# Two layers' matmuls as pairs of half-height products in one TensorE step

## The chip, the cores and the metric

The kernel runs on one core of one Trainium2 chip. The metric is the device time of one launch in microseconds (us), lower is better. TensorE is called PE (its weight loads PEld), VectorE DVE, ScalarE ACT, GpSimd POOL and SyncE SP.

## What is computed

A causal convolution over 7 taps per head (softmax of the taps first), then two feed-forward layers, each d_model 192, d_ff 2048, on 8192 tokens, float32 in and out.

```python
x = attn_out                                # conv of 7 taps over 2 x 4096 tokens, 192 channels
h = x @ w_in                                # layer 1
g = h * np.clip(h + 3.0, 0.0, 6.0) / 6.0
x = g @ w_out
h = x @ w_in2                               # layer 2
P = a[0] + a[1]*h + a[2]*h**2 + a[3]*h**3
Q = 1.0 + abs(b[0])*abs(h) + abs(b[1])*h**2
out = (P / (Q + 1e-6)) @ w_out2
```

## The kernel before

Tokens lie along the free dimension in 16 blocks of 512 (NB), d_ff in 16 tiles of 128 (NF), so each layer has 256 tiles (NT). To keep accuracy, each float32 operand is split in two fp32r parts, a rounded "hi" and a rest "lo". The 192 channels are kept as 128 (called a) and 64 (called b). Of b the hi and lo parts stand above each other in the 128 partitions of one tensor, `xb_hl`, so one matmul takes both.

**A tile's products.** `in_product` (line 359) makes h of one tile with five matmuls 128x512 into one PSUM bank: w_hi x a_hi, w_lo x a_hi, w_hi x a_lo, w_hi x b_hl, w_lo x b_hl. `out_product` (lines 371 to 377) adds one tile's g to the output sums with five: three into `ya_acc` (y0a_acc for layer 1, y1a_acc for layer 2 in the profile), then two into `yb_acc`, whose 128 rows hold the products of w_out's b columns, hi and lo part.

**The step.** An order written out by hand drives every engine. `course` lists steps; at step p PE does in1 of tile p (layer 1), in2 of tile s (layer 2, 21 tiles behind), out1 of tile p-2 and out2 of tile s-4: twenty matmuls. The table MIDDLE, with the lag of each operation, says in what order each other engine issues. ACT has eight operations a step: relu1 (writes r, line 463), rec2 (h<-rsq), sq2 (sqr), abs2 (den), lin2 (num), g1hi (g_hi<-r), g2hi (g_hi<-g), rsq2 (rsq). DVE has six: num2 (num, line 509), num1 (num, line 514), g_neg (g, line 569), gate1 (r<-r,h, line 470), newton (den, line 540), g_first (line 547). POOL has three: den_sum, g1lo, g2lo.

**Banks.** Eight PSUM banks: four for h, one each for the ya and yb sums of the two layers. From step 20 on all tiles of layer 1 use one h bank and those of layer 2 take turns in the three others. `wait_bank` makes PE wait: in1(p) for gate1(p-1), in2(s) for the third tile before it.

**Work once per block of 16 tiles.** The convolution's taps for later blocks (DVE, `conv_a_tap`, `conv_b_tap`), their split, and the hand-over from sums to inputs: when out1 of a block's last tile is done (n1_done), ACT copies y0a_acc (y1a_out) and rounds yb (`x2b_hi`), DVE makes the rest (`x2b_res`) and adds it to the lower-part sums (`x2b_lo`, which writes xb_hl of layer 2). The first out1 of the next block waits with its ya matmuls for y1a_out and with its yb matmuls for x2b_lo. In layer 2 the same holds for y2a_out (ACT) and `y2b_sum` (DVE, after y2b_move on ACT), which write the results that SP stores.

Of the kernel before, what the change touches and what calls it, by code (L numbers as in the profile page):

```python
# [11 lines left out]
P = 128  # L12
# [10 lines left out]
SUMS_READY, TAPS_READY = 5, 4  # L23


IN2, OUT1 = 20, 2


EARLY = IN2 + 1
# [96 lines left out]
def build_program(nc, x_a, x_b, taps, coefs, w_pack, out):  # L126
# [3 lines left out]
    NF = n_chunks * WCHUNK  # L130
# [3 lines left out]
    NT = NB * NF  # L134
# [7 lines left out]

    course, p, s = [], -1, -1
    while s < NT + SUM2 - NF + 1:
        one = p < NT + SUM1 - NF + 1
        p += one
        two = p >= IN2
        s += two  # L150
        course.append((p, s, one, two))
        if one and p in EXTRA:
            s += 1
            course.append((p, s, False, True))
# [28 lines left out]
    with ExitStack() as ctx:  # L183
# [13 lines left out]
        WO = DA + P + DA  # L197
        wout = [sb(f"wout{l}", NF * WO, F32R) for l in range(2)]
        stage_w = [sb(f"stage_w{i}", pack_cols) for i in range(W_STAGES)]

# [95 lines left out]
        def wait_buffer(eng, t, used, *others):  # L296
# [20 lines left out]
        names = """h1_done relu1 gate1 g1hi g1lo n1_done  # L317
# [44 lines left out]
        def out_product(eng, l, t, g_hi, g_lo, left):  # L362

            k, f = divmod(t, NF)
            c = f * WO
            w = wout[l]
            first, last = f == 0, f == NF - 1
            a_hi, b_hl, a_lo = w[:, c:c + DA], w[:, c + DA:c + DA + P], w[:, c + DA + P:c + WO]
# [8 lines left out]
            return eng.matmul(yb_acc[l][:, :], b_hl, g_lo[:, :], start=False, stop=last)  # L377


        def pe_in1(eng, t):  # L380
            split = ("cs_a_hi", "cs_a_lo", "cs_b_lo")
            if t < H_BANKS:
# [9 lines left out]
                in_product(eng, 0, t, h1_of(t), split, rest).then_inc(S["h1_done"], 1)  # L392
                return
            first_block_weights(eng, 0, t, "w_in_done")
            wait_bank(eng, 0, t)
            in_product(eng, 0, t, h1_of(t), split).then_inc(S["h1_done"], 1)

        def pe_out1(eng, t):
            first_block_weights(eng, 0, t, "w_out_done")
            eng.wait_ge(S["g1lo"], t + 1)  # L400
            out_product(eng, 0, t, g1_hi[t % 2], g1_lo[t % 2], ("y1a_out", "x2b_lo")) \
                .then_inc(S["n1_done"], 1)

# [13 lines left out]
        def pe_out2(eng, t):  # L417
            first_block_weights(eng, 1, t, "w_out_done")
            if t == 0:
                eng.wait_ge(S["g1lo"], EARLY)  # L420
            if t in full:
# [206 lines left out]
        def x2b_hi(eng, k):  # L628
            eng.wait_ge(S["n1_done"], (k + 1) * NF)
            after(eng, S["h2_done"], (k - 1) * NF)  # L630
            round_hi(eng, xb_hl[1][k % 2][0:DB, :], yb_acc[0][0:DB, :]).then_inc(S["x2b_hi"], 1)

        def x2b_res(eng, k):
            eng.wait_ge(S["x2b_hi"], k + 1)
            eng.tensor_tensor(x2b_rest[DB:P, :], yb_acc[0][0:DB, :], f32(xb_hl[1][k % 2][0:DB, :]),
                              ALU.subtract).then_inc(S["x2b_res"], 1)

        def x2b_lo(eng, k):
            eng.wait_ge(S["x2b_res"], k + 1)
            eng.tensor_tensor(xb_hl[1][k % 2][DB:P, :], x2b_rest[DB:P, :], yb_acc[0][DB:P, :],  # L640
                              ALU.add).then_inc(S["x2b_lo"], 1)


# [479 lines left out]
```

## Time and profile before

| | us |
|---|---|
| median of 2 runs | 1202.91 |
| profiled execution, time | 1202.42 |
| profiled execution, span of the instructions | 1200.3 |
| PE busy | 1185.5 |
| ACT busy | 1168.2 |
| DVE busy | 1157.7 |
| POOL busy | 1072.2 |
| PE weight loads busy | 962.9 |

Busy time is the union of an engine's instructions. Neighbouring instructions overlap at their ends, so an engine's rate is read from one start to the next. A row of the timeline gives start, duration, engine, line, operation, output <- inputs, shape, and in brackets idle time of the engine before it with what ended it.

### The profile page before, as it was taken

What the parts mean: (1) busy time and instruction counts of PE and PEld (TensorE: products, weight loads), DVE (VectorE), ACT (ScalarE), POOL (GpSimd) and SP (SyncE); (2) the same over time, 40 slices, a digit from 0 to 9 for tenths busy, and PEclk for the clock granted to TensorE, in tenths of its full rate; (3) what the DMA queues carried; (4) which work ended last, traced back from release to release, by engine and by line L of the source; (5) the groups of instructions that cost most, each with busy time, mean ns of one, the idle gap of its engine ahead of it and who ended that gap; (6) DMA issues with size and microseconds to landing.
All of it is one profiled execution on the core that took longest, in us unless ns stands there. A gap on an engine that the chain in (4) does not pass through costs nothing.

```text
span 1200.3 us, 18336 instructions
## 1 busy us (share of the span) xinstructions
PE 1185.5 (99%) x5145; PEld 962.9 (80%) x5145; DVE 1157.7 (96%) x1776; ACT 1168.2 (97%) x2235; POOL 1072.2 (89%) x829
## 2 busy tenths in 40 slices
PE   8999999999999999999999999999999999999988
PEld 6778888888888888888888888888888888888754
DVE  7899999999999999999999999999999999999898
ACT  8899999999999999999999999999999999999997
POOL 6889989999999989999899998999989999898875
PEclk9999999999999999999999999999999999999999
DMA  4400000000001000010000000000000000000010
GB/s 150 150 1 10 6 18 1 23 10 23 1 1 32 1 23 1 1 32 1 23 1 21 12 1 23 1 23 10 1 23 1 23 1 1 14 1 14 1 44 13
DMA packets 11317, 22.06 MB, mean 18 GB/s; under 512 B 1744, under 2 KB 3152, under 8 KB 11216
## 3 DMA queue, kind: packets, MB, share of 16 engines
q1 hardware_dynamic: 10928, 20.89, 5.9%
q8 instruction: 40, 0.66, 0.2%
q14 instruction: 61, 0.50, 0.1%
q10 hardware_dynamic: 288, 0.01, 0.0%
HBM read 14.60 MB, written 6.29 MB: 17 GB/s over the span
## 4 chain that ended last, share of the span: by engine, by line
PE 91%; ACT 4%; DVE 2%; issue 2%; POOL 0%; DMA 0%; ACTq 0%; DVEq 0%; POOLq 0%
PE h L359 45%; PE y0b_acc L376 5%; PE y0b_acc L377 5%; PE y0a_acc L371 5%; PE y0a_acc L373 5%; PE y0a_acc L372 5%; PE y1b_acc L377 4%; PE y1a_acc L373 4%; PE y1a_acc L371 4%; PE y1a_acc L372 4%; PE y1b_acc L376 4%; ACT rsq L524 0%; ACT g_hi L600 0%; ACT y0a_acc L536 0%; ACT num L491 0%
## 5 line engine op out<-in xcount | busy, mean ns | idle before, releaser
L520 POOL TENSOR_TENSOR den<-den,sqr 128x512 f32<-128x512 f32 x246 | 358.9, 1459 | 91.1 <-ACT den L497 90.1
L594 POOL TENSOR_TENSOR g_lo<-g,g_hi 128x512 fp32r<-128x512 f32 x246 | 321.7, 1308 | 5.3 <-ACT g_hi L600 5.3
L484 POOL TENSOR_TENSOR g_lo<-r,g_hi 128x512 fp32r<-128x512 f32 x235 | 306.9, 1306 | 5.5 <-ACT g_hi L600 3.6
L514 DVE SCALAR_TENSOR_TENSOR num<-num,coef,h 128x512 f32<-128x512 f32 x246 | 183.8, 747 | 8.3
L547 DVE SCALAR_TENSOR_TENSOR h<-num,coef,h 128x512 f32<-128x512 f32 x238 | 178.1, 748 | 0.2
L509 DVE TENSOR_TENSOR num<-num,h 128x512 f32<-128x512 f32 x246 | 167.8, 682 | 10.1 <-ACT num L491 3.9
L491 ACT ACTIVATE num<-h,coef 128x512 f32<-128x512 f32 x246 | 176.4, 717 | 0.2
L524 ACT ACTIVATE rsq<-den 128x512 f32<-128x512 f32 x246 | 159.0, 646 | 10.3 <-POOL den L520 7.2
L470 DVE SCALAR_TENSOR_TENSOR r<-r,h 128x512 f32<-128x512 f32 x235 | 160.7, 684 | 4.8 <-ACT r L463 3.7
L600 ACT ACTIVATE g_hi<-g 128x512 fp32r<-128x512 f32 x246 | 162.2, 659 | 2.4 <-DVE g L569 0.7
L540 DVE SCALAR_TENSOR_TENSOR den<-den,h 128x512 f32<-128x512 f32 x238 | 161.8, 680 | 0.6 <-ACT h L536 0.3
L569 DVE SCALAR_TENSOR_TENSOR g<-den,h 128x512 f32<-128x512 f32 x238 | 161.7, 679 | 0.2
L463 ACT ACTIVATE r<-h 128x512 f32<-128x512 f32 x256 | 154.4, 604 | 2.8 <-DVE y1b_acc L470 1.1
L600 ACT ACTIVATE g_hi<-r 128x512 fp32r<-128x512 f32 x235 | 156.3, 665 | 0.0
L497 ACT ACTIVATE den<-h 128x512 f32<-128x512 f32 x246 | 151.7, 617 | 1.7 <-DVE g L569 1.7
L503 ACT ACTIVATE sqr<-h 128x512 f32<-128x512 f32 x246 | 150.2, 610 | 0.6
L536 ACT ACTIVATE h<-rsq 128x512 f32<-128x512 f32 x240 | 147.4, 614 | 1.3
L371 PE MATMUL y0a_acc<-g_hi,wout 128*128 128x512 f32 x256 | 100.0, 390 | 2.2 <-DVE g_lo L484 1.6
L359 PE MATMUL h<-x0a_hi,win_hi 128*128 128x512 f32 x256 | 100.3, 392 | 1.1 <-DVE r L470 1.1
L359 PE MATMUL h<-x1a_hi,win_hi 128*128 128x512 f32 x256 | 100.5, 393 | 0.8 <-ACT x1a_hi L600 0.8
L359 PE MATMUL h<-x1a_lo,win_hi 128*128 128x512 f32 x256 | 99.7, 390 | 0.6 <-POOL x1a_lo L608 0.6
L359 PE MATMUL h<-x0a_lo,win_hi 128*128 128x512 f32 x256 | 99.6, 390 | 0.5 <-POOL win_lo L608 0.5
(177 smaller groups left out, 2995.9 us busy)
## 6 DMA issues: line engine op xcount, KB each, us to landing
stage_w<-w_pack SPq DMA_DIRECT2D x16, 448.0 KB, 3.3
raw_a<-x_a SPq DMA_DIRECT2D x16, 259.0 KB, 3.3
out<-y_a SPq DMA_DIRECT2D x16, 256.0 KB, 2.0
out<-y_b SPq DMA_DIRECT2D x16, 128.0 KB, 2.3
raw_b<-x_b SPq DMA_DIRECT2D x14, 129.5 KB, 2.7
r<-w_pack SPq DMA_DIRECT2D x4, 96.0 KB, 2.1
raw_b<-x_b SPq DMA_DIRECT2D x4, 65.5 KB, 4.7
y_a<-w_pack SPq DMA_DIRECT2D x2, 96.0 KB, 2.1
```

Of the source, the lines that this page charges most:

```text
L359: mm = eng.matmul(psum, w, x[:, :], start=(i == 0), stop=(i == len(passes) - 1))
L371: eng.matmul(ya_acc[l][:, :], a_hi, g_hi[:, :], start=first, stop=False)
L484: eng.tensor_tensor(g1_lo[t % 2][:, :], gated(t)[:, :], f32(g1_hi[t % 2][:, :]), ALU.subtract).then_inc(S["g1lo"], 1)
L491: eng.activation(num_of(t), h2_of(t), ACT.Identity, bias=a2, scale=reg_a3) \
L509: eng.tensor_tensor(n, n, h2_of(t), ALU.mult).then_inc(S["num2"], 1)
L514: eng.scalar_tensor_tensor(out=n, in0=n, scalar=a1, in1=h2_of(t), op0=ALU.add, op1=ALU.mult).then_inc(S["num1"], 1)
L520: eng.tensor_tensor(den_of(t), den_of(t), sqr_of(t), ALU.add).then_inc(S["den_sum"], 1)
L540: eng.scalar_tensor_tensor(out=den_of(t), in0=den_of(t), scalar=Q_ONE, in1=quotient(t), op0=ALU.add, op1=ALU.mult).then_inc(S["newton"], 1)
L547: eng.scalar_tensor_tensor(out=raw_quotient(t), in0=num_of(t), scalar=a0, in1=quotient(t), op0=ALU.add, op1=ALU.mult).then_inc(S["g_first" ...
L569: eng.scalar_tensor_tensor(out=g2[t % 2][:, :], in0=den_of(t), scalar=2.0, in1=raw_quotient(t), op0=ALU.subtract, op1=ALU.mult) \
L594: eng.tensor_tensor(g2_lo[t % 2][:, :], g2[t % 2][:, :], f32(g2_hi[t % 2][:, :]), ALU.subtract).then_inc(S["g2lo"], 1)
L600: return eng.activation(dst, src, ACT.Copy)
```

## The change

For the 232 steps that have tiles of both layers in full (p from 24 to 255), `pe_step` takes the place of the four calls. A matmul is cut in two halves of 64 contraction rows (partitions 0 to 63 and 64 to 127). `side_by_side` issues two halves behind each other that use different rows of the array and different banks: one of layer 1, one of layer 2. The groups follow one another: five pairs with layer 1's lower and layer 2's upper rows of the in products; the two yb pairs of the out products; four pairs with the in products' other rows (the fifth, w_lo x the b_lo rows of `xb_hl`, is not issued); three ya pairs; then the out products' other rows, two yb and three ya pairs. That is nineteen pairs. PE waits for its own earlier half before it writes the same bank from the other rows. Both layers' h are done behind the eleventh pair, both out products at the end of the step.

For the upper and lower rows to fit, layer 2's input b now holds its lo part in partitions 0 to 63 and hi in 64 to 127 (`x2b_hi`, `x2b_res`, `x2b_lo` write other partitions), and layer 1's w_out has its b columns first, lo before hi. For layer 1's odd blocks, whose `xb_hl` has hi in the upper rows, the product that is not issued is w_lo x b_hi. The orders of ACT, DVE, POOL and SP are what they were.

```diff
+        def side_by_side(eng, one, two, rows1, rows2, starts=(False, False), stops=(False, False)):
+            (out1, w1, x1), (out2, w2, x2) = one, two
+            return (eng.matmul(out1, w1[rows1, :], x1[rows1, :], start=starts[0], stop=stops[0]),
+                    eng.matmul(out2, w2[rows2, :], x2[rows2, :], start=starts[1], stop=stops[1]))
+        def pe_step(eng, p, s, n):
+            lower, upper = slice(0, DB), slice(DB, P)
+            t1, t2 = p - OUT1, s - OUT2
...
+            wait_bank(eng, 0, p)
+            wait_bank(eng, 1, s)
...
+                mm = side_by_side(eng, one, two, lower, upper, (i == 0, i == 0))
+            mm[0].then_inc(S["h1_part"], 1)
+            mm[1].then_inc(S["h2_part"], 1)
+
+            eng.wait_ge(S["g1lo"], t1 + 1)
+            eng.wait_ge(S["g2lo"], t2 + 1)
+            eng.wait_ge(S["n1_done"], t1)
+            after(eng, S["n2_done"], t2)
...
+            mm = first_rows((3, 4), ("x2b_lo", "y2b_sum"))
+            mm[0].then_inc(S["y1b_part"], 1)
+            mm[1].then_inc(S["y2b_half"], 1)
+
+            eng.wait_ge(S["h1_part"], n)
+            eng.wait_ge(S["h2_part"], n)
+            for i, (one, two) in enumerate(ins[:4]):
+                mm = side_by_side(eng, one, two, upper, lower, stops=(i == 3, i == 3))
+            mm[0].then_inc(S["h1_done"], 1)
+            mm[1].then_inc(S["h2_done"], 1)
+
+            mm = first_rows((0, 1, 2), ("y1a_out", "y2a_out"))
+            mm[0].then_inc(S["y1a_part"], 1)
+            mm[1].then_inc(S["y2a_half"], 1)
+
+            eng.wait_ge(S["y1b_part"], n)
+            eng.wait_ge(S["y2b_half"], n)
+            for i in (3, 4):
+                side_by_side(eng, *outs[i], upper, lower, stops=lasts if i == 4 else never)
+            eng.wait_ge(S["y1a_part"], n)
+            eng.wait_ge(S["y2a_half"], n)
+            for i in (0, 1, 2):
+                mm = side_by_side(eng, *outs[i], upper, lower, stops=lasts if i == 2 else never)
+            mm[0].then_inc(S["n1_done"], 1)
+            mm[1].then_inc(S["n2_done"], 1)
...
-            round_hi(eng, xb_hl[1][k % 2][0:DB, :], yb_acc[0][0:DB, :]).then_inc(S["x2b_hi"], 1)
+            round_hi(eng, xb_hl[1][k % 2][DB:P, :], yb_acc[0][DB:P, :]).then_inc(S["x2b_hi"], 1)
...
+        if not packs:
+            o = np.concatenate([o[:, :, da:], o[:, :, :da]], axis=2)
```

The first place is PE's step up to the end of h1. Before (h is layer 1's bank with x0 inputs, layer 2's with x1), the middle of a step's in products:

```order
L359 MATMUL h<-x0b_hl,win_hi 128x512
L359 MATMUL h<-x0b_hl,win_lo 128x512
L359 MATMUL h<-x1a_hi,win_hi 128x512 [waits g_done]
L359 MATMUL h<-x1a_hi,win_lo 128x512
L359 MATMUL h<-x1a_lo,win_hi 128x512
```

h of layer 1 is complete with the second row, the fifth matmul of the step. Now, the pairs of the upper and lower rows with which both h are completed:

```order
L412 MATMUL h<-x0a_hi,win_hi 128x512 [waits h2_part,h1_part]
L413 MATMUL h<-x1a_hi,win_hi 128x512
L412 MATMUL h<-x0a_hi,win_lo 128x512
L413 MATMUL h<-x1a_hi,win_lo 128x512
L412 MATMUL h<-x0a_lo,win_hi 128x512
L413 MATMUL h<-x1a_lo,win_hi 128x512
L412 MATMUL h<-x0b_hl,win_hi 128x512
L413 MATMUL h<-x1b_hl,win_hi 128x512
L412 MATMUL y0a_acc<-g_hi,wout 128x512 [waits y1a_out]
```

These are the eighth to eleventh pair; h of layer 1 moved from the fifth matmul behind the eleventh pair.

The second place is PE at the first tile of a block of layer 1, the out product's waits. Before:

```order
L359 MATMUL h<-x1b_hl,win_hi 128x512
L359 MATMUL h<-x1b_hl,win_lo 128x512
L371 MATMUL y0a_acc<-g_hi,wout 128x512 [waits y1a_out,g1lo]
L372 MATMUL y0a_acc<-g_hi,wout 128x512
L373 MATMUL y0a_acc<-g_lo,wout 128x512
L376 MATMUL y0b_acc<-g_hi,wout 128x512 [waits x2b_lo]
L377 MATMUL y0b_acc<-g_lo,wout 128x512
```

The wait for x2b_lo stands thirteen matmuls into the step. Now:

```order
L412 MATMUL h<-x0b_hl,win_lo 128x512
L413 MATMUL h<-x1b_hl,win_lo 128x512
L412 MATMUL y0b_acc<-g_hi,wout 128x512 [waits n2_done,n1_done,x2b_lo,g2lo,g1lo]
L413 MATMUL y1b_acc<-g_hi,wout 128x512
L412 MATMUL y0b_acc<-g_lo,wout 128x512
L413 MATMUL y1b_acc<-g_lo,wout 128x512
L412 MATMUL h<-x0a_hi,win_hi 128x512 [waits h2_part,h1_part]
```

It stands five pairs into the step, ahead of the other half of both h. There are 14 such rows with x2b_lo, and 14 with y2b_sum in its place.

The third place is DVE at the same step, where x2b_lo (line 640) is released. It reads the same before and now, but for the line numbers:

```order
L547 SCALAR_TENSOR_TENSOR h<-num,coef,h 128x512 [waits rec]
L509 TENSOR_TENSOR num<-num,h 128x512 [waits sq2,lin2]
L635 TENSOR_TENSOR x2b_rest<-y0b_acc,x1b_hl 64x512 [waits x2b_hi]
L640 TENSOR_TENSOR x1b_hl<-x2b_rest,y0b_acc 64x512 [waits x2b_res]
L514 SCALAR_TENSOR_TENSOR num<-num,coef,h 128x512 [waits num2]
L569 SCALAR_TENSOR_TENSOR g_0<-den,h 128x512 [waits g2lo,g_first,newton]
L470 SCALAR_TENSOR_TENSOR r_0<-r_0,h 128x512 [waits relu1]
```

Nothing moved on DVE.

## Rows read from the trace of the kernel before

**Rows 1.** The page: span, busy time of the engines, chain that ended last

```profile
span 1200.3 us, 18336 instructions
...
PE 1185.5 (99%) x5145; PEld 962.9 (80%) x5145; DVE 1157.7 (96%) x1776; ACT 1168.2 (97%) x2235; POOL 1072.2 (89%) x829
...
PE 91%; ACT 4%; DVE 2%; issue 2%; POOL 0%; DMA 0%; ACTq 0%; DVEq 0%; POOLq 0%
```

**Rows 2.** Window 600 to 750: busy (xcount) of PE, PEld, DVE, ACT, POOL, clock, DMA

```profile
600.00:750.00 150.00, 150.00 (x663) 124.20 (x662) 147.54 (x226) 148.06 (x284) 137.62 (x104) 1.00 0.04 12
```

**Rows 3.** Timeline, a step without block work on ACT and DVE

```profile
340.91 0.68 DVE L470 SCALAR_TENSOR_TENSOR r<-r,h 128x512 f32<-128x512 f32 x1
...
341.03 0.58 ACT L503 ACTIVATE sqr<-h 128x512 f32<-128x512 f32 x1
...
344.11 0.60 ACT L463 ACTIVATE r<-h 128x512 f32<-128x512 f32 x1
...
344.75 0.69 DVE L470 SCALAR_TENSOR_TENSOR r<-r,h 128x512 f32<-128x512 f32 x1
...
345.11 0.61 ACT L503 ACTIVATE sqr<-h 128x512 f32<-128x512 f32 x1
```

**Rows 4.** Timeline, block work on ACT and one tap on DVE

```profile
338.35 0.62 ACT L614 ACTIVATE y_a<-y0a_acc 128x512 f32<-128x512 f32 x1
338.82 0.66 ACT L524 ACTIVATE rsq<-den 128x512 f32<-128x512 f32 x1
...
339.82 0.67 ACT L600 ACTIVATE x1a_hi<-y_a 128x512 fp32r<-128x512 f32 x1
340.49 0.60 ACT L536 ACTIVATE h<-rsq 128x512 f32<-128x512 f32 x1
...
640.40 0.74 DVE L700 SCALAR_TENSOR_TENSOR conv_a<-raw_a,tap,conv_a 128x512 f32<-128x512 f32 x1
641.06 0.75 DVE L547 SCALAR_TENSOR_TENSOR h<-num,coef,h 128x512 f32<-128x512 f32 x1
```

**Rows 5.** Timeline, PE's weight loads behind a wait and in the stream

```profile
17.80 0.19 PEld L371 LDWEIGHTS y0a_acc<-g_hi,wout 128*128 128x128 f32 x1 [1.25 <-POOL wout L608]
17.91 0.19 PEld L372 LDWEIGHTS y0a_acc<-g_hi,wout 128*128 128x128 f32 x1
...
337.06 0.19 PEld L359 LDWEIGHTS h<-x0a_hi,win_lo 128*128 128x128 f32 x1
...
341.65 0.19 PEld L359 LDWEIGHTS h<-x0a_hi,win_hi 128*128 128x128 f32 x1 [0.32 <-DVE r L470]
...
341.75 0.19 PEld L359 LDWEIGHTS h<-x0a_hi,win_lo 128*128 128x128 f32 x1
```

**Rows 6.** Timeline, first tile of a block of layer 1, from the gate before it

```profile
334.98 0.69 DVE L470 SCALAR_TENSOR_TENSOR r<-r,h 128x512 f32<-128x512 f32 x1
...
337.06 0.39 PE L359 MATMUL h<-x0a_hi,win_hi 128*128 128x512 f32 x1
...
337.35 0.61 ACT L600 ACTIVATE x1b_hl<-y0b_acc 64x512 fp32r<-64x512 f32 x1
...
338.21 0.68 DVE L635 TENSOR_TENSOR x2b_rest<-y0b_acc,x1b_hl 64x512 f32<-64x512 f32 x1
...
338.93 0.69 DVE L640 TENSOR_TENSOR x1b_hl<-x2b_rest,y0b_acc 64x512 fp32r<-64x512 f32 x1
...
340.00 0.39 PE L376 MATMUL y0b_acc<-g_hi,wout 128*128 128x512 f32 x1
```

**Rows 7.** Timeline, first tile of a block of layer 2, from the gate before it

```profile
362.35 0.68 DVE L470 SCALAR_TENSOR_TENSOR r<-r,h 128x512 f32<-128x512 f32 x1
...
364.46 0.39 PE L359 MATMUL h<-x0a_hi,win_hi 128*128 128x512 f32 x1
...
366.25 0.68 DVE L660 SCALAR_TENSOR_TENSOR y_b<-y1b_acc,y_b 64x512 f32<-64x512 f32 x1
...
368.54 0.39 PE L376 MATMUL y1b_acc<-g_hi,wout 128*128 128x512 f32 x1
```

More of the change, by code:

```diff
@@ L23 @@
 SUMS_READY, TAPS_READY = 5, 4
-IN2, OUT1 = 20, 2
+IN2, OUT1, OUT2 = 20, 2, 4
 EARLY = IN2 + 1
@@ L151, in build_program @@
         course.append((p, s, one, two))
+        if one and two and p < NT and s >= OUT2:
+            in1_both.add(p)
+            in2_both.add(s)
+            out1_both.add(p - OUT1)
+            out2_both[s - OUT2] = (p, s, len(out2_both) + 1)
         if one and p in EXTRA:
@@ L315, in build_program @@
         d_const, d_tap, d_out_a, d_out_b = (sem(n) for n in ("d_const", "d_tap", "d_out_a", "d_out_b"))
-        names = """h1_done relu1 gate1 g1hi g1lo n1_done
+        names = """h1_done h1_part h2_part y1a_part y1b_part y2a_half y2b_half relu1 gate1 g1hi g1lo n1_done
                    h2_done lin2 abs2 sq2 num2 num1 den_sum rsq_done rec newton g_first g_done less_two g_gpsimd
@@ L367, in out_product @@
             first, last = f == 0, f == NF - 1
[L368 removed]
+            a_hi, b_hl = w[:, c + OUT_A[l]:c + OUT_A[l] + DA], w[:, c + OUT_B[l]:c + OUT_B[l] + P]
+            a_lo = w[:, c + DA + P:c + WO]
             if first:
@@ L377, in out_product, with in_places @@
             return eng.matmul(yb_acc[l][:, :], b_hl, g_lo[:, :], start=False, stop=last)
+        def in_places(l, t, psum):
+            k, f = divmod(t, NF)
+            par, c = k % 2, f * 2 * P
+            hi, lo = win_hi[l], win_lo[l]
+            return [(psum, hi[:, c:c + P], xa_hi[l][par]), (psum, lo[:, c:c + P], xa_hi[l][par]),
+                    (psum, hi[:, c:c + P], xa_lo[l][par]), (psum, hi[:, c + P:c + 2 * P], xb_hl[l][par]),
+                    (psum, lo[:, c + P:c + 2 * P], xb_hl[l][par])]
@@ new lines, in pe_step, with first_rows @@
+        def pe_step(eng, p, s, n):
+            lower, upper = slice(0, DB), slice(DB, P)
+            t1, t2 = p - OUT1, s - OUT2
+            ins = list(zip(in_places(0, p, h1_of(p)), in_places(1, s, h2_of(s))))
+            outs = list(zip(out_places(0, t1, g1_hi[t1 % 2], g1_lo[t1 % 2]),
+                            out_places(1, t2, g2_hi[t2 % 2], g2_lo[t2 % 2])))
+            wait_bank(eng, 0, p)
+            wait_bank(eng, 1, s)
+            needs = {0: ("cs_a_hi", "x2a_hi"), 2: ("cs_a_lo", "x2a_lo"), 3: ("cs_b_lo", "x2b_lo")}
+            for i, (one, two) in enumerate(ins):
+                for t, name in zip((p, s), needs.get(i, ())):
+                    if t % NF == 0:
+                        eng.wait_ge(S[name], t // NF + 1)
+                mm = side_by_side(eng, one, two, lower, upper, (i == 0, i == 0))
[5 more added lines that the diff above has]
+            after(eng, S["n2_done"], t2)
+            starts, lasts = (t1 % NF == 0, t2 % NF == 0), (t1 % NF == NF - 1, t2 % NF == NF - 1)
+            never = (False, False)
+            def first_rows(part, left):
+                for i in part:
+                    for t, start, name in zip((t1, t2), starts, left):
+                        if start and i == part[0]:
+                            after(eng, S[name], t // NF)
+                    mm = side_by_side(eng, *outs[i], lower, upper, starts if i == part[0] else never)
+                return mm
+            mm = first_rows((3, 4), ("x2b_lo", "y2b_sum"))
[20 more added lines that the diff above has]
+            mm[1].then_inc(S["n2_done"], 1)
@@ L394, in pe_in1 @@
             first_block_weights(eng, 0, t, "w_in_done")
+            if t in in1_both:
+                return
             wait_bank(eng, 0, t)
@@ L399, in pe_out1 @@
             first_block_weights(eng, 0, t, "w_out_done")
+            if t in out1_both:
+                return
             eng.wait_ge(S["g1lo"], t + 1)
@@ L405, in pe_in2 @@
             first_block_weights(eng, 1, t, "w_in_done")
+            if t in in2_both:
+                return
             wait_bank(eng, 1, t)
@@ L420, in pe_out2 @@
                 eng.wait_ge(S["g1lo"], EARLY)
+            if t in out2_both:
+                pe_step(eng, *out2_both[t])
+                return
             if t in full:
```

21 lines of the change are left out of this document (16 added, 5 removed).

## The prediction

> **What bounds the kernel now.** The page's first part comes first [rows 1]: TensorE (PE) is busy 99%, ScalarE (ACT) 97%, VectorE (DVE) 96% of a span of 1200.3 us, and the chain of waits runs 91% over PE. The stretch 600 to 750 says the same of the middle: 663 matmuls in 150 us, so one per 226.6 ns, and a step of twenty in 4.53 us, with no idle PE [rows 2]. So PE is the bound, but how near are the others? A busy share hides that here, because neighbouring instructions overlap; I read from start to start. The timeline of 341 to 346 us holds a step without block work: ACT's eight operations take 4.08 us from one sqr to the next, DVE's six 3.84 us from one r to the next [rows 3]. To that comes the work done once per block of 16 steps, priced by the start of the next instruction: some 8.5 operations of ACT at 0.47 to 0.67 us (4.6 us), and some 13 of DVE at 0.66 to 0.72 (8.7 us) [rows 4, 6]. That makes 4.08 + 4.6/16 = 4.37 us of ACT and 3.84 + 8.7/16 = 4.38 us of DVE per step. Both have only 3% less to do than PE. The profiled execution took 1202.42 us (1200.3 us and 2.1 around it), the median of the runs is 1202.91, the same thing; I sum against 1202.4.
>
> **What the change takes from PE.** 232 steps (those with tiles of both layers) go from 20 full matmuls to 38 half ones in 19 pairs; the rest of the program, 505 matmuls, stays. If a pair costs what one matmul costs, a step takes 19 x 0.2266 = 4.31 us, 0.23 less, and 52 us could go in all. The trace has no matmul on half of the rows, so I bound the pair. From below: 226.6 ns, since both halves stream 512 columns. From above: both halves one after the other, 453 ns. What could hold it between is the weight load, of which a pair has two. A load lasts 188 ns, but the second of two starts 0.11 us after the first where nothing holds it [rows 5], so two take 0.22 us of the load path and just fit into 0.2266. I take 226.6 ns as the nearest row, without margin: 0.24 is easily possible.
>
> A load starts as the matmul before it starts, in the same rows of the array (337.06 both) [rows 5, 6], so it loads under a running matmul. Next to that stands a rule. The Trainium skill ("TensorE: Matmul & The Clock Gate", Part 3, What overlaps and what doesn't) says that a weight load overlaps matmuls in flight only when its row group differs. By that rule each half would take its load and its matmul in turn; the trace of the full array disagrees, and what it would cost is part of rival (c).
>
> **The loop through the single h bank of layer 1.** h1 of step p+1 may start only when gate1(p) is done. Before, h1 is finished by the fifth of twenty matmuls; now by the eleventh of nineteen pairs (the order rows of the first place). Counted from a step's first matmul T: the eleventh starts at T + 2.27, ends 0.39 later [rows 6], and with 0.04 for the signal (as between relu1's end and gate1 [rows 3]) relu1 starts at T + 2.70. gate1 starts 0.64 after relu1 and takes 0.68, the first weight load follows 0.06 after it and the next one, with which the stream is under way, 0.11 after that [rows 3, 5]. The sum is 4.19 us, under 4.31, so the loop alone does not bind. But its slack has gone from over 1.2 us to 0.12: before, gate1 ends 1.39 us ahead of the next step (334.98 + 0.69 against 337.06) [rows 6]; now at most 0.3. Before, that slack lets ACT and DVE be late by a block operation and catch up. Now a step is about the largest of PE's 4.31, ACT's 4.08 and DVE's 3.84, each with its own block work in that very step. DVE with one tap has 4.50, ACT with one block operation 4.6. For the 14 of 16 steps that are not boundaries (below) this gives 4.50 us where nothing is evened out, and 4.33 where all is. I take 4.45, nearer to the first: 0.08 less than now, over 204 steps -17 us.
>
> **The waits at the block's boundary.** This is the step that decides. PE's out product of the first tile of a block may not overwrite y0b_acc before DVE's x2b_lo has read it, nor y1b_acc before y2b_sum. Before, the yb product stands after the ya product, thirteen matmuls into the step (layer 1) and eighteen (layer 2). In the change the yb pairs come first, right behind five pairs, at T + 1.13 (order rows, second place). In the trace x2b_lo ends at 338.93 + 0.69 = 339.62, T + 2.56, with T = 337.06 and PE needing it at 340.00 [rows 6]. y2b_sum ends at 366.25 + 0.68 = 366.92, T + 2.46, needed at 368.54, T + 4.08 [rows 7]. ACT's and DVE's order is unchanged (the order rows of the third place stand so in both), so even with the phase of before PE would stop 1.4 us. And the phase moves: gate1(p-1) ended 1.39 and 1.43 us ahead of T, now 0.17 to 0.3, so DVE stands some 1.15 us later against PE [rows 6, 7]. The release comes at T + 3.7. Then PE has to load (0.17), run the two yb pairs and the four upper pairs (the last starts 1.13 later), and the loop goes on: relu1 1.74 us after the release, gate1 at 2.38, the next step at 3.23. The step lasts 3.7 + 3.2 = 6.9 us in place of 4.53. The order shows 14 such places for x2b_lo and 14 for y2b_sum: 28 x 2.37 = +66 us. What covers nothing here: the second halves of h1 and h2 stand behind the waiting yb pair, and relu1, gate1, sq2 behind these. The floor of such a release is what hangs on n1_done: the last matmul of the step before ends at about T + 0.2, then x2b_hi 0.61, x2b_res 0.68, x2b_lo 0.69, T + 2.3 [rows 6]; then the step would be 5.5 us.
>
> **Edits with no price.** PE's waits for its own sums (h1_part, y1b_part, y1a_part) keep the two halves of one bank apart. Two of the three stand two pairs behind what they wait for: a matmul ends 0.39 after its start, signal and load make 0.17 of it more, 0.56, and the next pair is due at 0.68, so with the second half starting 0.11 late nothing is left. I put them at zero; if they show, 0.1 each, twice in 232 steps, +46 us at most, less where PE waits for gate1 anyway. x2b's swapped rows are the same instructions on DVE and ACT, and the weights' new order costs one different slice. g1lo and g2lo are needed 1.2 and 2.3 us earlier in the step and have two and four steps of lag.
>
> **Sum.** 1202.4 - 17 + 66 = 1252 us.
>
> **Rivals.**
> (a) Faster, or even: the boundary costs its floor and all else is evened out. 28 x 0.97 = +27, 204 x 0.20 = -41: 1188 us. To be over 2% faster the boundary would have to cost nothing, against [rows 6]. For it: the stop lets ACT and DVE work off what they are behind with. Over 2% faster 0.04, within 2% (up to 1227, boundary at its floor and the rest near 4.45) 0.13.
> (b) A pair costs more than one matmul: 0.25 us, by two loads of 0.11 and the 0.03 that lies between a matmul's start and the end of the load's turn. PE's step is 4.75, the loop 4.4: 204 x 0.25 = +51, 28 x 2.8 = +78: 1331 us. Chance 0.12. The Trainium skill ("TensorE: Matmul & The Clock Gate", Part 3) gives 3.07 times for four row tiles in place of four; that speaks for a pair dearer than one matmul, and no row here shows it.
> (c) The halves are not side by side (the change does not do what it says): 38 x 0.2266 = 8.61 us, 232 x 4.08 = +946, 2150 us. A load that waits for its own rows' matmul (0.11 + 0.39 = 0.50 us per pair) is dearer still: 19 x 0.50 = 9.5 us, 2355 us. Chance of both 0.05. The second is what the page's rule on row groups above would give.
> (d) The clock: PE would stand still 2.7 us in 28 places; the granted clock is 1.00 in the middle [rows 2], and the longest stop before, once PE runs, is 1.25 us [rows 5]. If it fell from 2.4 to 1.2 GHz after each stop and the next 4 us (my guess) went at half the rate, 28 x 2 = +56: 1308 us. Chance 0.06.
>
> **Numbers.** The forecast's own case has 0.60. The predicted time is 1252. The range goes from 1212 (shift of the phase half as large, the rest at 4.40) to 1290 (pairs of 0.24 us or the own waits showing): it leaves out (c), most of (b) and (d), and the good end of (a). 2% is about what a measurement tells from no change: under 1179 faster, over 1227 slower. Faster 0.05, within 14%, slower 0.81.
>
> **What the next profile would show.** Right: PE's time per pair 0.227 from start to start; 28 steps of nearly 7 us, with PE waiting over 2 us for x1b_hl and y_b of DVE; a few tenths of waiting for DVE's r in most other steps; DVE and ACT busy shares down to 92 to 94%. Wrong: pairs of 0.24 or more (b), no overlap of the two halves (c), a clock under 1.00 (d), or a wait for y_b under 1.5 us (a). What would upset the whole is a wait that PE has on itself and that I priced at nothing.

## The result and the profile after

The changed kernel takes 1303.44 us (median of 2 runs, 1302.61 to 1304.28) against 1202.91: 1.084 times the time of before, 95% interval 1.079 to 1.088. The prediction had the direction and the main mechanism, 1252 us and a range up to 1290; the loss is 100 us where it had 49. The profiled execution took 1304.28 us, 101.9 more than that of before.

The page of the changed kernel, its span, busy line, chain shares and three groups (name and shape, xcount | busy, mean ns | idle before, releaser):

```profile
span 1302.2 us, 28016 instructions
...
PE 1201.0 (92%) x9321; PEld 996.0 (76%) x9321; DVE 1167.4 (90%) x1776; ACT 1183.6 (91%) x2235; POOL 1071.0 (82%) x829
...
DVE 31%; PE 31%; ACT 22%; issue 14%; POOL 1%; ACTq 0%; DMA 0%; DVEq 0%; POOLq 0%
...
L412 PE MATMUL y0b_acc<-g_hi,wout 64*128 64x512 f32 x464 | 186.2, 401 | 70.4 <-DVE y_b L766 35.5
L576 DVE SCALAR_TENSOR_TENSOR r<-r,h 128x512 f32<-128x512 f32 x235 | 161.2, 686 | 88.3 <-ACT r L569 86.5
L569 ACT ACTIVATE r<-h 128x512 f32<-128x512 f32 x256 | 153.0, 598 | 86.9 <-PE h L412 78.5
```

Against [rows 1], the chain is no longer one engine's: PE's share has gone from 91% to 31%, and DVE, ACT and issue hold the rest. That is the picture of a loop that passes through three engines. PE stands idle 70.4 us in front of the first yb pair, and gate1 (DVE, line 576) and relu1 (ACT, line 569) wait in their turn, since the second halves of h stand behind that pair.

The windows of the changed kernel (columns as in [rows 2]): the middle, and then four of 2 us around one stop.

```profile
600.00:750.00 150.00, 137.75 (x1148) 113.99 (x1146) 136.49 (x208) 137.49 (x260) 126.92 (x95) 0.98 0.05 12
122.00:124.00 2.00, 0.05 (x2) 0.08 (x2) 1.94 (x4) 1.95 (x4) 2.00 (x3) 1.00 0.00 0
124.00:126.00 2.00, 2.00 (x12) 1.87 (x14) 1.06 (x2) 0.13 (x1) 0.72 (x1) 0.64 0.00 0
126.00:128.00 2.00, 2.00 (x12) 1.83 (x12) 0.69 (x1) 1.57 (x4) 0.38 (x1) 0.51 0.00 0
128.00:130.00 2.00, 2.00 (x21) 1.96 (x19) 1.71 (x3) 2.00 (x5) 1.81 (x2) 1.00 0.00 0
```

PE is idle from 122 to 124, and then the granted clock, the last column but two, reads 0.64 and 0.51: PE is at its lower level, 1.2 GHz in place of 2.4, for about 3.4 us in all, and a window of 2 us holds 12 half matmuls instead of 21. ACT and DVE are busy for only 1.7 and 1.75 us of these 4, since they wait for PE, so this time is lost to the whole loop. Before, no stretch up to PE's last matmul reads under 1.00. Counted in windows of 2 us, the changed kernel has 21 such stretches: behind all 14 waits for y2b_sum, behind 6 of the 14 for x2b_lo, and one at 1240, in the last part.

The pairs, from PE's timeline of the changed kernel, with the load of one (rows in order of start):

```profile
603.97 0.39 PE L413 MATMUL h<-x1a_hi,win_lo 64*128 64x512 f32 x1
...
604.03 0.39 PE L412 MATMUL h<-x0a_hi,win_lo 64*128 64x512 f32 x1
604.03 0.18 PEld L412 LDWEIGHTS h<-x0a_lo,win_hi 64*128 64x128 f32 x1
604.21 0.39 PE L413 MATMUL h<-x1a_lo,win_hi 64*128 64x512 f32 x1
...
604.26 0.39 PE L412 MATMUL h<-x0a_lo,win_hi 64*128 64x512 f32 x1
...
604.43 0.39 PE L413 MATMUL h<-x1b_hl,win_hi 64*128 64x512 f32 x1
```

Two halves start 0.06 us apart, the next two 0.23 later: a pair costs one full matmul. The load of 604.03 runs under a matmul of layer 1 that occupies the same 64 rows, so in this kernel too a load overlaps a matmul of its own row group. The Trainium skill ("TensorE: Matmul & The Clock Gate", Part 3, What overlaps and what doesn't) says that a load overlaps matmuls in flight only when its row group differs; these rows disagree with it.

**The step lengths**, from the first matmul of one step to that of the next, account for the loss; values for several steps are means. The description of the step gives layer 2 a lag of 21 tiles; it is 20 up to step 235 and 19 after it, which only says which steps hold the waits for y2b_sum.

| steps of the 232 | before | after | difference, us |
|---|---|---|---|
| 14 with the wait for x2b_lo | 4.53 | 7.12 at full clock | +36 |
| 14 with the wait for y2b_sum | 4.53 | 7.30 at full clock (from e2 and e4) | +39 |
| the clock, 20 of these 28 | | 8.66 for 7.12, 8.79 for 7.30 | +30 |
| 13 with p = 15 modulo 16 | 4.53 | 5.60 (5.34 to 5.95) | +14 |
| step 235 | 6.80 | 7.96 | +1 |
| the other 190 | 4.54 | 4.43 | -20 |
| sum | | | +100 of 101.9 |

One boundary, ACT's and DVE's timeline of the changed kernel (the step starts at T = 200.82, the one before it at 196.49):

```profile
199.22 0.60 ACT L569 ACTIVATE r<-h 128x512 f32<-128x512 f32 x1
...
201.76 0.65 ACT L706 ACTIVATE g_hi<-r 128x512 fp32r<-128x512 f32 x1
202.37 0.68 DVE L615 TENSOR_TENSOR num<-num,h 128x512 f32<-128x512 f32 x1
202.43 0.59 ACT L706 ACTIVATE x1b_hl<-y0b_acc 64x512 fp32r<-64x512 f32 x1
203.08 0.69 DVE L741 TENSOR_TENSOR x2b_rest<-y0b_acc,x1b_hl 64x512 f32<-64x512 f32 x1
203.81 0.68 DVE L746 TENSOR_TENSOR x1b_hl<-x2b_rest,y0b_acc 64x512 fp32r<-64x512 f32 x1
204.63 0.46 PE L412 MATMUL y0b_acc<-g_hi,wout 64*128 64x512 f32 x1 [2.48 <-DVE x1b_hl L746]
206.32 0.60 ACT L569 ACTIVATE r<-h 128x512 f32<-128x512 f32 x1 [1.50 <-PE h L412]
```

relu1 starts 2.73 us after its step (forecast 2.70), x2b_lo ends at T + 3.67 (forecast 3.7), the step lasts 7.12 (forecast 6.9). And the stretch at half clock, PE's timeline behind the stop that ends at 123.95:

```profile
124.84 0.62 PE L413 MATMUL h<-x1a_hi,win_lo 64*128 64x512 f32 x1
...
125.27 0.62 PE L413 MATMUL h<-x1a_lo,win_hi 64*128 64x512 f32 x1
...
125.70 0.62 PE L413 MATMUL h<-x1b_hl,win_hi 64*128 64x512 f32 x1
```

Pairs are 0.43 us apart there. What relu1 waits for comes later by it, so the whole loop does.

PE's waits in the changed kernel, 300 to 900 (total us, times, longest):

```profile
PEld y0b_acc L412 <- POOL g_lo L590: 44.0, 15, 3.0
...
PEld h L412 <- DVE r L576: 25.2, 56, 1.6
PE y0b_acc L412 <- DVE y_b L766: 20.4, 8, 2.6
PE y0b_acc L412 <- DVE x1b_hl L746: 17.5, 7, 2.5
```

The first row is the same 15 stops, seen by the load queue; the wait holds five semaphores, and g_lo had long been there. It is the last two rows that name the cause. The second is the loop through the single h bank: 56 short waits for gate1, where the kernel before had 0.6 us of them in all.

### The profile page after: what moved, and what is told of

The parts are those of the page before. It is cut to its first block, busy times and chain, and to the rows that moved or that the text cites. A ratio compares the mean times of both kernels' runs of the same rounds, so it can differ in the third digit from the quotient of the medians.

```text
span 1302.2 us, 28016 instructions
## 1 busy us (share of the span) xinstructions
PE 1201.0 (92%) x9321; PEld 996.0 (76%) x9321; DVE 1167.4 (90%) x1776; ACT 1183.6 (91%) x2235; POOL 1071.0 (82%) x829
## 3 DMA queue, kind: packets, MB, share of 16 engines
q8 instruction: 78, 1.28, 0.4%
## 4 chain that ended last, share of the span: by engine, by line
DVE 31%; PE 31%; ACT 22%; issue 14%; POOL 1%; ACTq 0%; DMA 0%; DVEq 0%; POOLq 0%
PE h L413 7%; PE h L412 7%; DVE num L615 6%; DVE g L675 5%; DVE r L576 5%; ACT num L597 4%; PE y0b_acc L412 4%; DVE h L653 4%; PE y0a_acc L412 3%; DVE conv_a L806 3%; PE y1a_acc L413 3%; ACT sqr L609 3%; ACT g_hi L706 3%; PE y1b_acc L413 2%; ACT rsq L630 2%
## 5 line engine op out<-in xcount | busy, mean ns | idle before, releaser
L412 PE MATMUL y0a_acc<-g_hi,wout 64*128 64x512 f32 x928 | 296.7, 400 | 0.0
L413 PE MATMUL y1a_acc<-g_hi,wout 64*128 64x512 f32 x928 | 296.7, 400 | 0.0
L412 PE MATMUL y0b_acc<-g_hi,wout 64*128 64x512 f32 x464 | 186.2, 401 | 70.4 <-DVE y_b L766 35.5
L412 PE MATMUL h<-x0a_hi,win_hi 64*128 64x512 f32 x464 | 192.8, 415 | 16.2 <-DVE r L576 14.2
L413 PE MATMUL h<-x1a_hi,win_hi 64*128 64x512 f32 x464 | 192.7, 415 | 0.0
L413 PE MATMUL y1b_acc<-g_hi,wout 64*128 64x512 f32 x464 | 187.2, 403 | 0.0
L412 PE MATMUL h<-x0b_hl,win_hi 64*128 64x512 f32 x464 | 184.7, 398 | 0.0
L413 PE MATMUL y1b_acc<-g_lo,wout 64*128 64x512 f32 x464 | 184.3, 397 | 0.0
L412 PE MATMUL y0b_acc<-g_lo,wout 64*128 64x512 f32 x464 | 184.3, 397 | 0.0
L412 PE MATMUL h<-x0a_lo,win_hi 64*128 64x512 f32 x464 | 184.1, 397 | 0.1
```

Source lines behind the costliest of these rows:

```text
L412: return (eng.matmul(out1, w1[rows1, :], x1[rows1, :], start=starts[0], stop=stops[0]), eng.matmul(out2, w2[rows2, :], x2[rows2, :], start ...
L413: eng.matmul(out2, w2[rows2, :], x2[rows2, :], start=starts[1], stop=stops[1]))
```

## The experiments

The kernel before took 1202.5 to 1203.1 us beside all of them. e5, e11 and e12 have four runs each, the others one; since the four runs of e11 lie 7 us apart (all of the kernel before under 1), a small difference of a changed kernel's single run counts only where the step lengths of its trace show it too.

**e1_rows_only** keeps the new layout (x2b's rows, the weights' order) without paired steps.

```diff
-        if one and two and p < NT and s >= OUT2:
+        if False and one and two and p < NT and s >= OUT2:
```

> The change's data layout alone (layer 2's input b with its low part first, layer 1's output weights with b first), no paired step: all steps are the twenty full matmuls of before. Theory: the layout costs nothing and all that was lost lies in the paired step, so 1203 us, within 3. Rival: the swapped rows on VectorE or the new weight order cost something at the block's hand-over; then 1206 us or more, with a new wait for x1b_hl or win/wout in the trace.

1206.61 us, as the rival said. ACT at a boundary of e1_rows_only:

```profile
337.46 0.70 ACT L706 ACTIVATE g_hi<-r 128x512 fp32r<-128x512 f32 x1
338.19 0.59 ACT L706 ACTIVATE x1b_hl<-y0b_acc 64x512 fp32r<-64x512 f32 x1
338.81 0.64 ACT L706 ACTIVATE g_hi<-g 128x512 fp32r<-128x512 f32 x1
339.47 0.60 ACT L720 ACTIVATE y_a<-y0a_acc 128x512 f32<-128x512 f32 x1
...
340.21 0.47 PE L383 MATMUL y0a_acc<-g_hi,wout 128*128 128x512 f32 x1 [0.33 <-ACT y_a L720]
```

The same copy on the other 64 partitions starts 0.73 us after its neighbour and holds the next for 0.62; in [rows 6] y_a's copy comes 1.00 after it [rows 4, 6], here 1.28. PE then waits for y_a: eight of the 14 boundary steps of x2b last 4.78 to 5.15 us, the other six 4.55 to 4.57, against 4.55 on average before. That is 3.4 us, nearly all of the 4. The new layout costs it, by what ACT's rows show through the swapped partitions. Why they hold the engine longer stays open.

**e2_fill** issues the five lower pairs of the in products twice in the 28 boundary steps (and in step 24, which has no wait), so that PE stands still 1.13 us less in each.

```diff
+            again = t1 % NF == 0 or t2 % NF == 0
...
+            if again:
+                for i, (one, two) in enumerate(ins):
+                    mm = side_by_side(eng, one, two, lower, upper, (i == 0, i == 0))
```

> The changed kernel, but in the 28 steps in which a block's first out product waits, TensorE issues the five lower-row pairs of the in products twice (the second time from a cleared bank, so the sums are the same). It shortens each stop from 2.5 us to about 1.4 us with work that is thrown away, and leaves what ends the stop where it is. Theory: the stops of about 2.5 us let the granted clock fall to half in 21 of 28 places, each worth 1.6 us; with stops of 1.4 us no stretch at half clock is left and the time is 1303 - 34 = 1269 us, with mean clock above 0.99. Rival: the fall of the clock costs nothing on the path (VectorE and ScalarE would be late anyway); then 1303 or slightly more.

1276.62 us, and no clock under 1.00 in the boundary steps: the stops last 1.1 to 1.4 us, the steps 7.07 (x2b) and 7.26 (y2b), as long as at full clock before. More work on PE, and 27 us less. The clock is what this takes away, 20 stretches at some 1.5 us being 30 us; the ordinary steps are 2 to 3 us longer in all (4.45).

**e3_late_sums** puts the wait back near its old place: in boundary steps the yb pairs come behind the ya pairs.

```diff
+            late = starts[0] or starts[1]
+            if not late:
+                yb_first()
...
+            if late:
+                yb_first()
```

> The changed kernel, but in the 28 steps with a block's first out product the groups stand in another order: both halves of the in products first, then the ya pairs, then the yb pairs, so that the wait for x2b_lo or y2b_sum comes at 2.9 us of the step in place of 1.13 and both h are finished ahead of it. Theory (the boundary wait blocks h, relu and gate behind it): these steps fall from 7.1 to 8.8 us to about 5.4, no stretch of half clock is left; 28 x (8.3 - 5.4) = 81 us less, 1222 us. Rival (the engines are late at the boundary in any case, and the place of the wait matters little): the wait moves to y_a or y_b at the new place with the same 2.5 us; 1265 us or more.

1235.93 us, 68 less, and no boundary step has half clock any more. Boundary steps come to some 5.9 us, not 5.4: the wait passes to the next in line, ACT's y_a, which stands behind x2b_hi. The waits of e3_late_sums, 300 to 900:

```profile
PEld y0a_acc L412 <- ACT y_a L738: 9.7, 8, 1.2
...
PEld y0a_acc L412 <- ACT y_a L774: 8.2, 8, 1.2
```

**e4_twenty** issues all five pairs of the second group, twenty in place of nineteen.

```diff
-            for i, (one, two) in enumerate(ins[:4]):
-                mm = side_by_side(eng, one, two, upper, lower, stops=(i == 3, i == 3))
+            for i, (one, two) in enumerate(ins):
+                mm = side_by_side(eng, one, two, upper, lower, stops=(i == 4, i == 4))
```

> The changed kernel with twenty pairs in a step in place of nineteen (the fifth in pair of the other rows is issued too). Theory (the steps between the boundaries are set by TensorE's pairs, or by the loop h1, relu1, gate1 with hardly any slack): a pair of 0.227 us more in each of 232 steps shows in nearly all of them, +40 to +53 us, 1350 us. Rival (ScalarE and VectorE with their own 4.38 us set these steps): the light steps grow by 0.1 to 0.2 only and the heavy ones not at all, +15 us, 1318 us.

1335.61 us, +32, between the two. The 190 ordinary steps go from 4.43 to 4.60 on average: of a pair's 0.227, 0.17 arrives. The loop through PE binds in most steps, though not in all. Half clock follows 20 stops here too, but others: 13 of 14 for x2b_lo and 7 of 14 for y2b_sum, and the other seven of these steps last 7.30 to 7.33.

**e6_full_at_first** issues the 28 boundary steps as full matmuls, in the order of before.

```diff
-        if one and two and p < NT and s >= OUT2:
+        if one and two and p < NT and s >= OUT2 and (p - OUT1) % NF and (s - OUT2) % NF:
```

> The changed kernel, with paired steps everywhere but in the 28 steps that hold a block's first out product; those go back to the twenty full matmuls in the order of before, where the ya wait comes at 2.3 us, the yb waits at 2.9 and 4.1 us and h of layer 1 is finished after five matmuls. Theory (the paired step loses at the boundary by where it waits and by what stands behind the wait): these steps fall to about 5.3 us, limited by VectorE and ScalarE with their block work, no stretch at half clock: 1303 - 28 x (8.3 - 5.3) = 1219 us. Rival (the change between full and half matmuls empties the array and costs 0.3 us or more, 56 times): 1236 us or more.

1233.55 us, 70 less, and still 30 over before. The boundary steps last 5.9 (x2b) and 5.1 (y2b), although their order is that of before (with the new layout). The phase differs: DVE and ACT come into them late, and PE, ten matmuls in, waits 0.9 for y_a. In e6_full_at_first, 300 to 900:

```profile
PE y0a_acc L383 <- ACT y_a L720: 7.1, 8, 0.9
```

Part of the 30 us is something else, the change between full matmuls and pairs, which the next run shows.

**e5_light_steps** pairs only the steps whose ACT and DVE have least to do, 89 of 232.

```diff
+        if one and two and p < NT and s >= OUT2 and p % NF in (3, 9, 10, 11, 12, 13):
```

> Paired steps only where p modulo 16 is 3 or 9 to 13, some 87 of 232 steps, which have little block work on VectorE and ScalarE; all others, the boundary steps among them, are twenty full matmuls as before. Theory (a pair costs 0.227 us like a matmul, and what the paired step lacks is the 1.2 us of slack between gate1 and the next step, which the full steps give back): each paired step is worth 0.1 to 0.2 us, with 4 us lost by the new layout: 1193 us, 0.992 of before. Rival (the slack taken in the paired steps is missing at the boundary and with VectorE's taps, and is paid there in full): 1206 us or more.

1217.71 us (1.012 times before, 1.011 to 1.014): slower, as the rival said, but only in part for its reason. The 89 paired steps save at most 20 us, and there are 60 changes between full matmuls and pairs. Each costs time by itself, as PE's rows of e5_light_steps show, first into pairs, then out of them:

```profile
345.78 0.39 PE L389 MATMUL y1b_acc<-g_lo,wout 128*128 128x512 f32 x1
346.10 0.49 PE L412 MATMUL h<-x0a_hi,win_hi 64*128 64x512 f32 x1
346.43 0.39 PE L412 MATMUL h<-x0a_hi,win_lo 64*128 64x512 f32 x1
...
350.34 0.39 PE L412 MATMUL y0a_acc<-g_lo,wout 64*128 64x512 f32 x1
350.66 0.50 PE L370 MATMUL h<-x0a_hi,win_hi 128*128 128x512 f32 x1
351.00 0.39 PE L370 MATMUL h<-x0a_hi,win_lo 128*128 128x512 f32 x1
```

The two starts behind a change come 0.32 to 0.34 us after the one before them in place of 0.227, in both directions: 0.2 us each, 12 us in all, in e6 as well. The layout is another 4. What is left, some 19 us by this count, is waits: paired steps last, by their place in the block, 4.31 to 4.56 in place of 4.31, and the boundary steps of x2b 5.25 on average (4.80 in e1). That part is the cushion of the steps that follow, as the rival has it.

**e7_after_no_taps** and **e8_before_no_taps** leave six of the seven taps of the convolution's 128 a channels out, in blocks 2 to 15, of the changed kernel and of the one before.

```diff
+            if k > 1 and j > 0:
+                return
...
-            ins.then_inc(S["conv_a_tap"], 1)
+            ins.then_inc(S["conv_a_tap"], K if k > 1 else 1)
```

> The changed kernel without VectorE's six further taps of the convolution's a part in blocks 2 to 15 (the first tap on ScalarE stays; so blocks 2 to 15 are computed from one tap of the 128 a channels only). It takes six of the some thirteen block operations off VectorE, 0.66 us each, 84 in all. Theory (in the change nothing evens out a late engine, because gate1 ends only 0.2 us ahead of the next step): the steps with a tap fall from 4.50 to about 4.35, and the release at both kinds of boundary, which has a tap of VectorE ahead of it, comes 0.66 us earlier, so the stops fall to about 1.9 us and the clock stays up: 14 x 5 x 0.15 = -10, 28 x 0.66 = -18, -34 for the clock: 1241 us. Rival (TensorE and its pairs set the steps, and the boundary hangs on n1_done alone): under 15 us less, 1290 us or more.

> The kernel before with the same taps left out (blocks 2 to 15 are computed from one tap of the a channels only). Theory: TensorE sets every step there and the taps lie beside it, so the time stays: 1202 us, at most 3 less. Rival (before too VectorE is at the bound): 10 us less or more.

1288.11 us (-15) and 1201.21 (-1.6). Of the 15, x2b_lo has nothing: it ends at T + 3.64 as before. The rows of e7_after_no_taps say why:

```profile
201.38 0.59 ACT L706 ACTIVATE x1b_hl<-y0b_acc 64x512 fp32r<-64x512 f32 x1
202.01 0.69 DVE L741 TENSOR_TENSOR x2b_rest<-y0b_acc,x1b_hl 64x512 f32<-64x512 f32 x1 [0.45 <-ACT x1b_hl L706]
```

DVE now waits for ACT: the release hangs on the place of x2b_hi in ACT's order. In the changed kernel both come at once: at T = 200.82, num2 ends at T + 2.23 on DVE and x2b_hi at T + 2.20 on ACT. y2b_sum ends 0.4 earlier (14 x 0.42 = 6 us), and five clock stretches fewer give 8. The 190 ordinary steps gain 2 us together, nearly all of it in two places, p = 6 and 7 modulo 16 in every other block (4.43 and 4.50 to 4.32 and 4.33). So the taps of the a channels are not what makes the mean step 4.43. The taps of the b channels stayed in, and their steps are as long as they were. The kernel before gains next to nothing, as its theory had it.

**e9_early** takes the hand-over forward in both orders, before lin2 on ACT and before num2 on DVE.

```diff
+             ("x2b_hi", SUM1, -1), ("y2b_move", SUM2, -1), ("lin2", 0), ("cs_a_hi", AHEAD, 10), ("g1hi", 0),
...
+    "vector": [("x2b_res", SUM1, 0), ("x2b_lo", SUM1, 0), ("y2b_sum", SUM2, 0), ("num2", 1), ("num1", 1),
```

> The changed kernel with the hand-over of the yb sums issued earlier by ScalarE and VectorE: x2b_hi and y2b_move stand ahead of lin2 in ScalarE's order, x2b_res, x2b_lo and y2b_sum ahead of num2 in VectorE's. TensorE's order is unchanged. Theory (the release at a boundary hangs on ScalarE's and VectorE's own order, in which x2b_hi only starts 1.6 us after the step does although n1_done has come at 0.2): the releases come at about 2.9 and 2.5 us of the step in place of 3.67 and 3.84, the stops shrink to 1.7 and 1.3 us and the clock stays up: 14 x 0.8 + 14 x 1.3 = -29, -34 for the clock: 1240 us. Rival (one operation earlier is another later, and lin2 and num2 are what the next gate waits for): the stops shrink and the steps behind them grow, 1265 us or more.

1252.87 us, 51 less. The releases move to T + 3.08 and T + 2.46, and the stops shrink with them. The waits of e9_early, 300 to 900:

```profile
PE y0b_acc L413 <- DVE x1b_hl L747: 15.2, 8, 1.9
PE y0b_acc L413 <- DVE y_b L767: 9.4, 8, 1.2
```

Behind stops of 1.2 us the clock holds in all 14; behind those of 1.9 it fell in 5 of 14 (8.1 against 6.5 us of step). The gain lies between what theory and rival had.

**e10_early_late** joins e3 and e9 and moves y1a_out and y2a_out forward too.

> The two cures together: the late place of the first sums in TensorE's boundary steps (as in the run with late sums) and the early hand-over, here with y1a_out and y2a_out too ahead of lin2. Theory: the wait of 0.8 to 1.2 us for y_a that was left in the boundary steps goes, they take 4.9 us in place of 5.85: 1236 - 28 x 0.95 = 1209 us, still above before, since the rest of the paired steps is at 4.42 with 5.55 once a block. Rival (the boundary steps are now set by ScalarE's 5.2 and VectorE's 5.3 us): 1225 us or more.

1228.82 us, the time that the rival had. The wait for y_a did go, as the theory said (no stop over 0.3 us is left in these steps), but they come to 5.7 and 5.2 us, not 4.9. No version with paired steps comes down to 1203.

**e11_split_later** is about the 13 steps of 5.6 us. In the changed kernel, a stretch with p = 15 modulo 16:

```profile
267.90 1.31 POOL L590 TENSOR_TENSOR g_lo<-r,g_hi 128x512 fp32r<-128x512 f32 x1
267.97 1.78 DVE L712 SCALAR_TENSOR_TENSOR x0b_hl<-conv_b,x0b_hl 64x512 fp32r<-64x512 f32 x1
...
271.12 0.50 PE L412 MATMUL h<-x0a_hi,win_hi 64*128 64x512 f32 x1 [1.23 <-DVE r L576]
```

A DVE operation that should take 0.7 takes 1.78, and PE pays 1.23 for it. So it is in the seven even blocks; in the six odd ones, where the step lasts 5.4, it is a tap of the b channels, 1.72. The first one is moved on DVE, from behind num1 to behind newton, where no POOL operation has just begun.

```diff
-             ("cs_b_lo", AHEAD, 15, 0), ("y2b_sum", SUM2, 0), ("g_neg", 2), ("gate1", 0), ("newton", 1),
+             ("y2b_sum", SUM2, 0), ("g_neg", 2), ("gate1", 0), ("newton", 1), ("cs_b_lo", AHEAD, 15, 0),
```

> The changed kernel with one DVE operation moved: the lower part of the convolution's b channels in even blocks (x0b_hl, 64x512, once in 32 steps) is issued behind newton instead of behind num1. Everything it reads and writes is in SBUF. In the changed kernel it lasts 1.78 us where POOL is in its g_lo operations throughout, and the steps of that place (tile 15 of a block) last 5.7 to 5.95 us instead of 4.4. Theory: it is long because POOL is in an operation on SBUF at the same time; behind newton POOL stands idle for about a microsecond, so it lasts about 0.75 us, the seven steps come down to 4.6 at most, and the time falls by 7 x 1.2 = 8 us, to 1295. The other places with tile 15 (odd blocks, 5.4 us, the long operation there is a tap) stay. Rival: the length belongs to the operation or its tensors (64 partitions, rounding output): it stays at 1.8 us wherever it stands, and the time stays at 1303.

1304.75 us (1299.45 to 1306.77, 4 runs): no gain, but the operation did what the theory says. In e11_split_later:

```profile
271.06 0.69 DVE L712 SCALAR_TENSOR_TENSOR x0b_hl<-conv_b,x0b_hl 64x512 fp32r<-64x512 f32 x1
...
271.80 0.50 PE L412 MATMUL h<-x0b_hl,win_hi 64*128 64x512 f32 x1 [0.35 <-DVE x0b_hl L712]
```

0.69 us, and the seven steps fall from 5.77 to 4.55 (-8.6). Two things take it back: the next step reads x0b_hl sooner than it now comes (4.46 to 5.06, +4), and the clock fell behind 26 boundary stops instead of 20 (+9). The stops for x2b_lo are no longer than before, 2.40 to 2.51 us against 2.42 to 2.51.

**e12_fill_and_later** joins e2's and e11's edits, to have the move without the clock.

> Both edits at once: in the 28 boundary steps the five lower pairs of the in products are issued twice (as in the run that did that alone, 1276.6 us), and the lower part of the convolution's b channels in even blocks stands behind newton on DVE (as in the run that did that alone, 1304.8 us). Theory: the move alone took 1.22 us out of seven steps and put 0.62 into the seven that follow, -4 us, and lost this because the granted clock then fell behind 27 stops instead of 21, for a reason that is not in the length of the stops (2.47 to 2.51 us in both). With the stops shortened by the repeated pairs no clock falls, and the -4 us show: 1272. Rival: something else in the moved order lengthens the boundary steps, and the time is 1276.6 or more; the x2b_lo steps would then not be the 7.06 us of the run with the repeated pairs alone.

1271.37 us (1270.80 to 1272.93, 4 runs) against 1276.62 (one run): the theory. (The counts of 27 and 21 in its expectation are 26 and 20 for the boundary stops.) The steps of x2b_lo last 7.09, the seven steps 4.51. So a repair worth 5 us at steady clock was invisible in e11, where six more stops were followed by half clock. Why more of them were stays open.

## Why the prediction was right or wrong

**What the change takes from PE: right.** A pair costs 0.227 us, which rejects (b) and (c). The rule of the Trainium skill beside (c) had a load wait for matmuls of its own rows, and here it does not.

**The loop through the single h bank: right in place and size, its carrier less so.** relu1 at T + 2.73 for 2.70, ordinary steps of 4.43 for 4.45, and e4 shows three quarters of one more pair arriving. "DVE with one tap has 4.50" as the term that fills the steps is borne out in a few places only: e7 without the a channels' taps keeps a mean of 4.42. Which of the loop's links adds the 0.1 over PE's 4.31 was not separated.

**The waits at the boundary: right.** Forecast +66, measured +75 at full clock, 7.12 and 7.30 us for 6.9. The release was foreseen to 0.03 (x2b_lo) and 0.14 us (y2b_sum, T + 3.84). The reason given, that DVE's phase decides, holds for y2b_sum; for x2b_lo ACT's order gives the same time even where DVE is early (e7), and e9, which moves both, gains 51 us.

**The step that failed** is rival (d), the clock: "Chance 0.06", and left out of the range. The prediction itself computed stops of 2.7 us, more than twice the longest of before (1.25), and priced the clock behind them at +56 if it fell each time. It fell in 20 of 28, and each time cost some 1.5 us, not 2: +30 in the boundary steps. e2 shows it as the cause: stops shortened by repeated work, 27 us back, and at 1277 us a time inside the range. With the clock the forecast would have been 1252 + 30 = 1282. A mechanism for which the trace of before has no row at all, and on which every one of the main term's stops depends, is an open cost that belongs into the range, not a rival at 0.06.

**The term that was missing** is +14 from the 13 steps with p = 15. The prediction took DVE's block operations at 0.66 to 0.72 each [rows 4, 6]. One per block is not, and the trace of the kernel before has it too, in the rows of its lines 606 (even blocks) and 715 (odd ones; xcount: minimum, median and maximum in ns):

```profile
L606 DVE SCALAR_TENSOR_TENSOR x0b_hl<-conv_b,x0b_hl x16: 418/687/1846, 39.7 to 1030.6; 64x512 fp32r<-64x512 f32 x14, 64x256 fp32r<-64x256 f32 x2
L715 DVE SCALAR_TENSOR_TENSOR conv_b<-raw_b,tap,conv_b x48: 480/745/1728, 18.8 to 967.0; 128x512 f32<-128x512 f32 x42, 128x256 f32<-128x256 f32 x6
```

There the slack of 1.39 us hid the longest of them. The prediction said that this slack goes to 0.12, and then did not look for single operations that exceed the median by more.

**Edits with no price: half right.** PE's waits for its own sums do not show: in boundary steps at full clock the pairs follow each other by 0.23 across them. "x2b's swapped rows are the same instructions" was wrong by 4 us (e1).

With the clock's 30 and the 14, the rest of the difference is +9 on the boundary waits, -3 on the ordinary steps and +1 for step 235: 1252 + 51 = 1303.

Two sums of the prediction do not come out, and neither bears on the outcome. The conditions of the range's lower end (28 x 1.8 = +50, 204 x 0.13 = -27) give 1226 us, not 1212. In (b), 4.75 less 4.53 is 0.22, so 45 in place of 51 and 1325 us.

## What to carry to other kernels

Busy shares say nothing of how much an edit may close a loop: count, for each buffer that a step hands back, the time from its release to its next use, and compare that with the longest single operation in the loop, not with the mean. A wait that moves forward in an in-order queue costs what stands behind it too, here the other halves of both h, and giving it its old place back (e3) or filling the stop with work (e2) are worth 68 and 27 us. Pairs in some steps only have a price of their own: each change between pairs and full matmuls cost 0.2 us here (e5). Where an edit makes TensorE stand still longer than it ever did in the profile, put the half clock behind each stop into the range.

## What the runs showed of the hardware

- **The clock.** Granted clock fell to half, for about 3.4 us, behind all 14 stops for y2b_sum (2.25 to 2.56 us), behind 6 of 14 for x2b_lo (2.42 to 2.51), behind 13 of 14 of these in e11 at the same length, behind only 7 of 14 stops for y2b_sum in e4 (2.28 to 2.48), and behind 5 of 14 of 1.9 us in e9; never behind the stops of 1.2 us there, nor behind those of 1.1 to 1.4 in e2. The length alone does not decide it.
- **Halves side by side.** Matmuls of 64 rows, 512 columns, in different rows and banks, run in pairs every 0.227 us through 232 steps, with both loads hidden. A change from full matmuls to pairs or back costs 0.2 us: the two starts behind it come 0.32 to 0.34 us after the one before them (e5, e6).
- **DVE beside POOL.** A DVE operation with all operands in SBUF that starts 0.07 us after a POOL operation lasts 1.78 us instead of 0.69 (e11), and the POOL operation behind it 1.73 instead of 1.30. In e11 the same operation starts 0.22 us ahead of one of POOL: it keeps its 0.69, and POOL's lasts 1.62. The Trainium skill ("SBUF — State Buffer", Who interferes with whom) says that a DVE instruction with two SBUF inputs contends with a GpSimd instruction that reads SBUF; the trace agrees: both of this one's tensor inputs are in SBUF, and it ends 0.54 us after POOL's first one does. The operations of DVE that read PSUM keep 0.67 to 0.76 beside a busy POOL.
- **ACT on the upper partitions.** With the 64x512 copy out of PSUM on partitions 64 to 127, the three starts from g_hi's to y_a's take 2.01 us (337.46 to 339.47 in e1), 0.5 more than with the copy on 0 to 63. The copy and the two operations behind it then start 0.03 us after the end of the one before, and not 0.13 to 0.17 ahead of it.
